# Layer 2's out-product with its operands swapped, tokens interleaved by four, and the coefficient set-up placed later

## The chip, the cores and the metric

The program runs on one core of one Trainium2 chip. The metric is the time of the device for one execution in microseconds, as the median of several; lower is better. The core has five engines that run their own instruction queues: TensorE (PE; its weight loads are listed apart as PEld), VectorE (DVE), ScalarE (ACT), GpSimd (POOL) and SyncE (SP), which issues most of the DMAs here.

## What is computed

A causal 7-tap filter over the sequence, and then two layers on 8192 tokens of 192 features, each with 2048 hidden units. The first has a relu6 gate, the second a rational activation.

```python
# x (2, 4096, 192); weight (8, 7); softmax over the taps of each head
out = np.einsum('hk,bskhg->bshg', softmax(weight), x_unf)      # filter
h = x @ w_in                                                   # layer 1
g = h * np.clip(h + 3.0, 0.0, 6.0) / 6.0
x = g @ w_out
h = x @ w_in                                                   # layer 2
P = a[0] + a[1] * h + a[2] * h2 + a[3] * h3
Q = 1.0 + np.abs(b[0]) * np.abs(h) + np.abs(b[1]) * h2
g = P / (Q + 1e-06)
return (g @ w_out).astype(np.float32)
```

## The kernel before

**Tiling.** Tokens are taken in 16 blocks (NB) of 512 (BLK), hidden units in 16 tiles of 128 (NF), which makes 256 tile steps (NT) per layer. Activations lie with features on the partitions: 192 features are a part "a" of 128 (DA) and a part "b" of 64 (DB). A tile step of a layer is an in-product (five matmuls that give h, 128 hidden units x 512 tokens, in one PSUM bank), elementwise work on VectorE, ScalarE and GpSimd that gives g, and an out-product (five matmuls that add g's share to the accumulators of the block).

**Split operands.** Matmuls use the rounded one-pass format fp32r. Every operand is held as a rounded high part and the rest, and a product is three: hi x hi, lo x hi, hi x lo. In `out_product` (L369 to 385) the weights w_out are the stationary operand and g the moving one with 512 columns: a_hi and a_lo on g_hi, a_hi on g_lo into `ya_acc` (L379 to 381), and a mixed operand b_hl, whose columns 0 to 63 are b's high part and 64 to 127 its low part, on g_hi and g_lo into `yb_acc` (L384, L385). Output rows are features, and `yb_acc` holds two halves that are added later.

**Order.** Every engine's queue is written out by `run` from hand-made plans (START, BEGIN, RAMP, MIDDLE, TURN, END): an entry is a stage, its lag in steps behind layer 1's step p or layer 2's step s, and for work of a block the step inside the block. Layer 2 starts 20 steps behind layer 1 (IN2). In the middle, a step has one layer-1 and one layer-2 tile, and TensorE's order is in1, in2, out1, out2.

**The end of a block in layer 2.** ScalarE scales `ya_acc` into `y_a` (y2a_out, L657) and the upper half of `yb_acc` into `y_b` (y2b_move, L664); VectorE adds the scaled lower half (y2b_sum, L669, for the last block also L675). The first out-product of the next block waits for these (`left` in `out_product`). `store_y` issues two DMAs, 256 and 128 KB, to an output laid out as features x batch x tokens; the host transposes it.

**The last tiles.** Nine of the last fifteen tiles (FULL) aren't split: their g and weights are plain fp32 (L433 and L434, two fp32 products that appear as two instructions each). Their weights, `w_full`, are loaded again by `load_w_full` from within `store_y` of block 14 into buffers that are no longer used. `spare_products` (L423) issues products whose result isn't used. From tile 236 on (DEEP) elementwise buffers are four deep and use, among others, columns 0 to 511 of `stage_w`.

**Set-up.** The activation is evaluated in a form that divides by the cubic coefficient. Eight VectorE operations on one column (`monic_...`, L949 to L978) prepare its constants; the START plan puts them behind layer 1's tiles 5 to 11, on VectorE's queue. The first num2 waits for all of them (MONIC_READY). Two PSUM banks of layer 2's accumulators serve as the buffer of layer 1's gate for the first 21 tiles (`gated`). WARM products on a tile of ones run before the first data is there (L1066).

Of the kernel before, what the change touches and what calls it, by code (L numbers as in the profile page):

```python
# [5 lines left out]
F32 = mybir.dt.float32  # L6
# [5 lines left out]
P = 128  # L12
# [37 lines left out]
    "vector": [("monic_side", 5), ("monic_safe", 6), ("monic_inverse", 7), ("monic_c2", 8), ("gate1", 0), ("monic_ratio", 9),  # L50
             ("monic_c01", 10), ("monic_scale", 11), ("conv_b1", AHEAD, (2, 2, 2, 3, 5, 6, 7), 1), ("g1lo", 1),
# [10 lines left out]
             ("x2b_res", SUM1, 0), ("g1lo", 1), ("x2b_lo", SUM1, 0), ("conv_a", AHEAD, (6, 4, 4, 16, 4, 5))],  # L62
# [15 lines left out]
    "scalar": [("y2b_move", SUM2, 0), ("y2a_out", SUM2, 0), ("cs_b_hi", AHEAD, 13, 0),  # L78
# [5 lines left out]
             ("cs_b_lo", AHEAD, 15, 0), ("y2b_sum", SUM2, 0), ("g_neg", 2), ("gate1", 0), ("newton", 1),  # L84
# [10 lines left out]
             ("y2b_move", SUM2, -3)],  # L95
    "vector": [("num2", 1), ("g_neg", 2), ("num1", 1), ("x2b_lo", SUM1, 8), ("newton", 1), ("g_first", 1),
             ("x2b_res", SUM1, 3), ("g2lo", 2), ("y2b_sum", SUM2, -2)],
# [7 lines left out]
             ("y2b_move", SUM2, 3)],  # L105
    "vector": [("num2", 1), ("y2b_sum", SUM2, 0), ("num1", 1), ("g_neg", 2), ("x2b_res", SUM1, -3), ("g2lo", 6),
# [22 lines left out]
def build_program(nc, x_a, x_b, taps, coefs, w_pack, out):  # L129
# [10 lines left out]
    assert n_batch == 2 and n_layers == 2 and DA + DB == out.shape[0] and DB * 2 == P  # L140
# [45 lines left out]
    with ExitStack() as ctx:  # L186
# [13 lines left out]
        WO = DA + P + DA  # L200
# [12 lines left out]
        y_a = [sb(f"y{l}_a", BLK) for l in range(2)]  # L213
        y2_b = sb("y2_b", BLK, F32, DB)
# [40 lines left out]
        ya_acc = [bank(f"y{l}a_acc") for l in range(2)]  # L255
        yb_acc = [bank(f"y{l}b_acc") for l in range(2)]

        yb_last = h_banks[bank2[NT - H_BANKS]][0:DB, :]
# [7 lines left out]
        def quotient(t):  # L266
            return ([ya_acc[0], yb_acc[0]][t % 2] if t >= SPARE else h_banks[bank2[t]])[:, :]
# [4 lines left out]
        spent = [r1[0], r1[1], y_a[0], raw_a[1], x2b_rest]  # L272
        w_full = {t: spent[i // 2][:, i % 2 * (DA + DB):(i % 2 + 1) * (DA + DB)] for i, t in enumerate(full)}
# [30 lines left out]
        def wait_buffer(eng, t, used, *others):  # L304
# [8 lines left out]
            else:  # L313
                eng.wait_ge(S[used], t - 3)
                if used == "g_first" and t - 4 in on_gpsimd:
# [6 lines left out]
        d_w_full = sem("d_w_full")  # L322
# [7 lines left out]
                   y2b_part y1a_out x2a_hi x2b_hi x2b_res x2a_lo x2b_lo  # L330
                   y2a_out y2b_move y2b_sum product_a product_b sum_p sum_v setup_v setup_s root ones""".split()
# [38 lines left out]
        def out_product(eng, l, t, g_hi, g_lo, left):  # L370

            k, f = divmod(t, NF)
            c = f * WO
            w = wout[l]
            first, last = f == 0, f == NF - 1
            a_hi, b_hl, a_lo = w[:, c:c + DA], w[:, c + DA:c + DA + P], w[:, c + DA + P:c + WO]
            if first:
                after(eng, S[left[0]], k)
            eng.matmul(ya_acc[l][:, :], a_hi, g_hi[:, :], start=first, stop=False)  # L379
            eng.matmul(ya_acc[l][:, :], a_lo, g_hi[:, :], start=False, stop=False)  # L380
            eng.matmul(ya_acc[l][:, :], a_hi, g_lo[:, :], start=False, stop=last)
            if first:
                after(eng, S[left[1]], k)
            eng.matmul(yb_acc[l][:, :], b_hl, g_hi[:, :], start=first, stop=False)  # L384
            return eng.matmul(yb_acc[l][:, :], b_hl, g_lo[:, :], start=False, stop=last)  # L385
# [20 lines left out]
        def pe_out1(eng, t):  # L406
            first_block_weights(eng, 0, t, "w_out_done")
            eng.wait_ge(S["g1lo"], t + 1)
            out_product(eng, 0, t, g1_hi[t % 2], g1_lo[t % 2], ("y1a_out", "x2b_lo")) \
                .then_inc(S["n1_done"], 1)  # L410
# [768 lines left out]
```

## Time and profile before

| | |
|---|---|
| median of 3 runs | 1202.07 us (1201.59 to 1202.16) |
| the profiled execution | 1204.0 us, its span 1201.9 us |
| granted TensorE clock, mean | 0.998 |
| TensorE / its weight loads | busy 1186.5 us (99%) / 963.2 us (80%) |
| VectorE | busy 1160.7 us (97%) |
| ScalarE / GpSimd | busy 1065.5 us (89%) / 1072.9 us (89%) |
| DMA | 22.02 MB, 18 GB/s over the span |

The span runs from the first to the last instruction of the program. A busy share is the union of an engine's instructions. Matmuls overlap in the records, so that their busy time says little about their pace: what counts is the time from one start to the next. "Idle before" is the time in which the engine did nothing ahead of a group, with the engine that released it.

### The profile page before, as it was taken

The numbers are of one execution on the slowest core, as the hardware profiler recorded it, in microseconds if no ns is written. First come the engines' busy times: TensorE is split into PE (matmuls) and PEld (weight loads), VectorE is DVE, ScalarE is ACT, GpSimd is POOL, SyncE is SP. The second block draws the span as 40 slices with busy tenths as digits, with TensorE's granted clock in tenths as the row PEclk, the third lists the DMA queues.
The fourth block names the chain that finished last, engine by engine and source line by source line (L and its number), as shares of the span: only waits on it lengthen the run. The fifth ranks groups of instructions, "written<-read, shape, count | busy, mean of one in ns | idle before, by whom it ended". The sixth has DMA issues, their size and how long they took to land. (4 is left out here: it accounts for less than half of the span.)

```text
span 1201.9 us, 17842 instructions
## 1 busy us (share of the span) xinstructions
PE 1186.5 (99%) x5145; PEld 963.2 (80%) x5145; DVE 1160.7 (97%) x1784; ACT 1065.5 (89%) x1980; POOL 1072.9 (89%) x829
## 2 busy tenths in 40 slices
PE   8999999999999999999999999999999999999998
PEld 6778888888888888888888888888888888888754
DVE  7999999999999999999999999999999999998898
ACT  7888899898998988989998899889999899888886
POOL 5989989898998989999898998999989899898874
PEclk9999999999999999999999999999999999999999
DMA  4400000000000000010000000000000000000010
GB/s 147 152 2 10 1 23 1 23 10 23 1 1 24 9 23 1 1 32 1 22 1 15 17 2 23 1 23 10 1 23 1 23 1 1 14 1 14 1 44 13
DMA packets 11313, 22.02 MB, mean 18 GB/s; under 512 B 1744, under 2 KB 3152, under 8 KB 11216
## 3 DMA queue, kind: packets, MB, share of 16 engines
q1 hardware_dynamic: 10928, 20.89, 5.9%
q8 instruction: 40, 0.66, 0.2%
q14 instruction: 57, 0.47, 0.1%
q10 hardware_dynamic: 288, 0.01, 0.0%
HBM read 14.60 MB, written 6.29 MB: 17 GB/s over the span
## 5 line engine op out<-in xcount | busy, mean ns | idle before, releaser
L525 POOL TENSOR_TENSOR den<-den,sqr 128x512 f32<-128x512 f32 x246 | 360.7, 1466 | 92.3 <-ACT den L499 91.1
L599 POOL TENSOR_TENSOR g_lo<-g,g_hi 128x512 fp32r<-128x512 f32 x246 | 319.4, 1298 | 7.9 <-ACT g_hi L605 7.9
L492 POOL TENSOR_TENSOR g_lo<-r,g_hi 128x512 fp32r<-128x512 f32 x235 | 309.9, 1319 | 1.7 <-ACT g_hi L605 1.3
L605 ACT ACTIVATE g_hi<-g 128x512 fp32r<-128x512 f32 x246 | 155.9, 634 | 54.9 <-PE y1b_acc L385 47.1
L529 ACT ACTIVATE rsq<-den 128x512 f32<-128x512 f32 x246 | 155.0, 630 | 45.6 <-POOL den L525 42.7
L519 DVE SCALAR_TENSOR_TENSOR num<-h,monic,num 128x512 f32<-128x512 f32 x246 | 184.6, 751 | 8.2
L513 DVE SCALAR_TENSOR_TENSOR num<-h,monic,sqr 128x512 f32<-128x512 f32 x246 | 183.2, 745 | 0.0
L552 DVE SCALAR_TENSOR_TENSOR h<-num,monic,h 128x512 f32<-128x512 f32 x238 | 178.3, 749 | 0.2
L478 DVE SCALAR_TENSOR_TENSOR r<-r,h 128x512 f32<-128x512 f32 x235 | 160.4, 683 | 14.2 <-ACT r L471 13.4
L545 DVE SCALAR_TENSOR_TENSOR den<-den,h 128x512 f32<-128x512 f32 x238 | 161.9, 680 | 1.0 <-ACT h L541 0.9
L574 DVE SCALAR_TENSOR_TENSOR g<-den,h 128x512 f32<-128x512 f32 x238 | 161.1, 677 | 0.2
L605 ACT ACTIVATE g_hi<-r 128x512 fp32r<-128x512 f32 x235 | 149.3, 635 | 8.7 <-issue 0.3
L471 ACT ACTIVATE r<-h 128x512 f32<-128x512 f32 x256 | 150.0, 586 | 5.9 <-DVE y1b_acc L478 2.5
L505 ACT ACTIVATE sqr<-h 128x512 f32<-128x512 f32 x246 | 145.2, 590 | 2.3
L541 ACT ACTIVATE h<-rsq 128x512 f32<-128x512 f32 x240 | 143.2, 597 | 4.4 <-DVE num L519 3.5
L499 ACT ACTIVATE den<-h 128x512 f32<-128x512 f32 x246 | 146.1, 594 | 0.0
L367 PE MATMUL h<-x0a_hi,win_hi 128*128 128x512 f32 x256 | 100.5, 393 | 2.3 <-DVE r L478 1.2
L379 PE MATMUL y0a_acc<-g_hi,wout 128*128 128x512 f32 x256 | 100.3, 392 | 2.3 <-DVE g_lo L492 1.6
L367 PE MATMUL h<-x1a_hi,win_hi 128*128 128x512 f32 x256 | 100.6, 393 | 0.1
L367 PE MATMUL h<-x0b_hl,win_hi 128*128 128x512 f32 x256 | 100.5, 393 | 0.0
L367 PE MATMUL h<-x1a_lo,win_hi 128*128 128x512 f32 x256 | 99.9, 390 | 0.6 <-POOL x1a_lo L613 0.6
L367 PE MATMUL h<-x0a_lo,win_hi 128*128 128x512 f32 x256 | 99.8, 391 | 0.6 <-DVE x0a_lo L611 0.6
(182 smaller groups left out, 2886.8 us busy)
## 6 DMA issues: line engine op xcount, KB each, us to landing
stage_w<-w_pack SPq DMA_DIRECT2D x16, 448.0 KB, 3.4
raw_a<-x_a SPq DMA_DIRECT2D x16, 259.0 KB, 3.2
out<-y_a SPq DMA_DIRECT2D x16, 256.0 KB, 2.0
out<-y_b SPq DMA_DIRECT2D x16, 128.0 KB, 2.3
raw_b<-x_b SPq DMA_DIRECT2D x14, 129.5 KB, 2.7
r<-w_pack SPq DMA_DIRECT2D x4, 96.0 KB, 2.0
raw_b<-x_b SPq DMA_DIRECT2D x4, 65.5 KB, 4.6
y_a<-w_pack SPq DMA_DIRECT2D x2, 96.0 KB, 2.3
```

The source lines that it names most:

```text
L367: mm = eng.matmul(psum, w, x[:, :], start=(i == 0), stop=(i == len(passes) - 1))
L478: eng.scalar_tensor_tensor(out=gated(t)[:, :], in0=r1[t % 2][:, :], scalar=1.0, in1=h1_of(t), op0=ALU.min, op1=ALU.mult).then_inc(S["gate1 ...
L492: eng.tensor_tensor(g1_lo[t % 2][:, :], gated(t)[:, :], f32(g1_hi[t % 2][:, :]), ALU.subtract).then_inc(S["g1lo"], 1)
L513: eng.scalar_tensor_tensor(out=num_of(t), in0=h2_of(t), scalar=c2, in1=sqr_of(t), op0=ALU.add, op1=ALU.mult).then_inc(S["num2"], 1)
L519: eng.scalar_tensor_tensor(out=n, in0=h2_of(t), scalar=c1, in1=n, op0=ALU.mult, op1=ALU.add).then_inc(S["num1"], 1)
L525: eng.tensor_tensor(den_of(t), den_of(t), sqr_of(t), ALU.add).then_inc(S["den_sum"], 1)
L529: eng.activation(rsq[t % 2][:, :], den_of(t), ACT.Abs_reciprocal_sqrt, bias=Q_ONE).then_inc(S["rsq_done"], 1)
L545: eng.scalar_tensor_tensor(out=den_of(t), in0=den_of(t), scalar=Q_ONE, in1=quotient(t), op0=ALU.add, op1=ALU.mult).then_inc(S["newton"], 1)
L552: eng.scalar_tensor_tensor(out=raw_quotient(t), in0=num_of(t), scalar=c0, in1=quotient(t), op0=ALU.add, op1=ALU.mult).then_inc(S["g_first" ...
L574: eng.scalar_tensor_tensor(out=g2[t % 2][:, :], in0=den_of(t), scalar=2.0, in1=raw_quotient(t), op0=ALU.subtract, op1=ALU.mult) \
L599: eng.tensor_tensor(g2_lo[t % 2][:, :], g2[t % 2][:, :], f32(g2_hi[t % 2][:, :]), ALU.subtract).then_inc(S["g2lo"], 1)
L605: return eng.activation(dst, src, ACT.Copy)
```

## The change

Layer 1 stays as it is. In layer 2's out-product the operands change places: g is the stationary operand, in four groups of 128 tokens, and w_out the moving one with 192 columns (D), so that output rows are tokens. A group takes every fourth token of the block (`tokens(i)`), and so partition p holds the tokens 4p to 4p + 3; two groups share a PSUM bank. A tile has 12 matmuls: per group w_hi and w_lo on g_hi, and w_hi on g_lo. Unsplit tiles have four fp32 products. `wout[1]` now holds w_hi and w_lo side by side, 384 columns a tile as before. Each bank is emptied by one scaled copy of 128 x 384; y2b_sum and the addition of halves are gone, and for the last block the second copy is on VectorE. The output is laid out as batch x tokens x features, and a store's rows are two tokens, 1536 bytes. Six of the nine unsplit weights go to free columns of `stage_w` (512 to 895), and are loaded one block earlier. The eight set-up operations move from the START plan (steps 5 to 11) to the BEGIN plan (steps 12 to 18). num2 and g_neg wait for the same events in another order.

```diff
 START = {
-    "vector": [("monic_side", 5), ("monic_safe", 6), ("monic_inverse", 7), ("monic_c2", 8), ("gate1", 0), ("monic_ratio", 9),
-             ("monic_c01", 10), ("monic_scale", 11), ("conv_b1", AHEAD, (2, 2, 2, 3, 5, 6, 7), 1), ("g1lo", 1),
+    "vector": [("gate1", 0), ("conv_b1", AHEAD, (2, 2, 2, 3, 5, 6, 7), 1), ("g1lo", 1),
 BEGIN = {
-             ("x2b_res", SUM1, 0), ("g1lo", 1), ("x2b_lo", SUM1, 0), ("conv_a", AHEAD, (6, 4, 4, 16, 4, 5))],
+             ("x2b_res", SUM1, 0), ("g1lo", 1), ("x2b_lo", SUM1, 0), ("conv_a", AHEAD, (6, 4, 4, 16, 4, 5)),
+             ("monic_side", 12), ("monic_safe", 13), ("monic_inverse", 14), ("monic_c2", 15), ("monic_ratio", 16),
+             ("monic_c01", 17), ("monic_scale", 18)],
 MIDDLE = {
-    "scalar": [("y2b_move", SUM2, 0), ("y2a_out", SUM2, 0), ("cs_b_hi", AHEAD, 13, 0),
+    "scalar": [("y2b_out", SUM2, 0), ("y2a_out", SUM2, 0), ("cs_b_hi", AHEAD, 13, 0),
-             ("cs_b_lo", AHEAD, 15, 0), ("y2b_sum", SUM2, 0), ("g_neg", 2), ("gate1", 0), ("newton", 1),
+             ("cs_b_lo", AHEAD, 15, 0), ("g_neg", 2), ("gate1", 0), ("newton", 1),
...
-        spent = [r1[0], r1[1], y_a[0], raw_a[1], x2b_rest]
-        w_full = {t: spent[i // 2][:, i % 2 * (DA + DB):(i % 2 + 1) * (DA + DB)] for i, t in enumerate(full)}
+        spent = [st[:, BLK:BLK + 2 * D] for st in stage_w] + [r1[0], r1[1], y1_a, raw_a[1], x2b_rest]
+        w_full = {t: spent[i // 2][:, i % 2 * D:(i % 2 + 1) * D] for i, t in enumerate(full)}
+        in_stage = full[:2 * W_STAGES]
...
+        def tokens(i):
+            return slice(i, BLK, BLK // P)
+
+        def y2_of(i):
+            return y2_acc[i // 2][:, i % 2 * D:(i % 2 + 1) * D]
+
+        def out_product2_hi(eng, t):
+            k, f = divmod(t, NF)
+            w, g_hi = wout[1][:, f * WO:(f + 1) * WO], g2_hi[t % 2]
+            for i in range(BLK // P):
+                y, g = y2_of(i), g_hi[:, tokens(i)]
+                if f == 0 and i % 2 == 0:
+                    after(eng, S[("y2a_out", "y2b_out")[i // 2]], k)
+                eng.matmul(y, g, w[:, 0:D], start=f == 0 and i % 2 == 0, stop=False, skip_group_check=True)
+                eng.matmul(y, g, w[:, D:WO], start=False, stop=False, skip_group_check=True)
+
+        def out_product2_lo(eng, t, groups):
+            f = t % NF
+            for i in groups:
+                ins = eng.matmul(y2_of(i), g2_lo[t % 2][:, tokens(i)], wout[1][:, f * WO:f * WO + D],
+                                 start=False, stop=f == NF - 1, skip_group_check=True)
+            return ins
...
             if t in full:
-                eng.wait_ge(d_w_full, 16 * len(full))
                 wait_g(eng, t)
-                w, g = w_full[t], g2[t % 2][:, :]
-                eng.matmul(ya_acc[1][:, :], w[:, 0:DA], g, start=False, stop=False)
-                eng.matmul(yb_acc[1][0:DB, :], w[:, DA:DA + DB], g, start=False, stop=False) \
-                    .then_inc(S["n2_done"], 1)
+                if t in in_stage:
+                    eng.wait_ge(d_w_stage, 16 * len(in_stage))
+                else:
+                    eng.wait_ge(d_w_full, 16 * (len(full) - len(in_stage)))
+                for i in range(BLK // P):
+                    ins = eng.matmul(y2_of(i), g2[t % 2][:, tokens(i)], w_full[t], start=False, stop=False,
+                                     skip_group_check=True)
+                ins.then_inc(S["n2_done"], 1)
             if t < NT - 2:
                 eng.wait_ge(S["g2lo"], splits(t))
-                out_product(eng, 1, t, g2_hi[t % 2], g2_lo[t % 2], ("y2a_out", "y2b_sum")) \
-                    .then_inc(S["n2_done"], 1)
+                out_product2_hi(eng, t)
+                out_product2_lo(eng, t, range(4)).then_inc(S["n2_done"], 1)
...
+        def y2_half(half):
+            return y2[:, half * 2 * D:(half + 1) * 2 * D]
-            eng.activation(y_a[1][:, :], ya_acc[1][:, :], ACT.Copy, scale=minus_scale).then_inc(S["y2a_out"], 1)
+            eng.activation(y2_half(0), y2_acc[0][:, 0:2 * D], ACT.Copy, scale=minus_scale).then_inc(S["y2a_out"], 1)
...
-        def y2b_sum(eng, k):
+        def y2b_out(eng, k):
+            if (k == NB - 1) != (eng is nc.vector):
+                return
+            eng.wait_ge(S["n2_done"], (k + 1) * NF)
             after(eng, d_out_b, 16 * k)
+            scaled(eng, y2_half(1), y2_acc[1][:, 0:2 * D], minus_scale).then_inc(S["y2b_out"], 1)
...
         def w_out_lo(eng, c):
+            if c >= n_chunks:
+                minus(eng, wo[:, :, D:WO], raw_out, f32(wo[:, :, 0:D])).then_inc(S["w_out_done"], 1)
+                return
...
         def store_y(eng, k):
+            if k == NB - 3:
+                load_w_full(eng, in_stage, d_w_stage, ("w_in_done", 2 * n_chunks), ("w_out_done", 2 * n_chunks))
             if k == NB - 2:
-                load_w_full(eng)
+                load_w_full(eng, full[len(in_stage):], d_w_full, ("g1lo", NT), ("x2a_lo", NB),
+                            ("conv_a_tap", K * NB), ("x2b_lo", NB))
+            rows = out[k % 2, bass.ds(k // 2 * BLK, BLK), :].rearrange("(p g) d -> p g d", p=P)
+            for half, name, landed in ((0, "y2a_out", d_out_a), (1, "y2b_out", d_out_b)):
+                eng.wait_ge(S[name], k + 1)
+                eng.dma_start(rows[:, 2 * half:2 * half + 2, :],
+                              y2_half(half).rearrange("p (g d) -> p g d", d=D)).then_inc(landed, 16)
```

## Rows read from the trace of the kernel before

**Rows 1.** The page's first part: busy time, share of the span, instructions.
```profile
PE 1186.5 (99%) x5145; PEld 963.2 (80%) x5145; DVE 1160.7 (97%) x1784; ACT 1065.5 (89%) x1980; POOL 1072.9 (89%) x829
```
**Rows 2.** Stages: length, then PE, PEld, DVE, ACT, POOL busy, clock, DMA share, GB/s.
```profile
100.00:1139.00 1039.00, 1039.00 (x4584) 860.36 (x4583) 1013.29 (x1550) 934.38 (x1724) 953.82 (x717) 1.00 0.04 11
...
1139.00:1202.00 63.00, 55.46 (x184) 30.51 (x182) 58.84 (x91) 47.34 (x88) 40.23 (x32) 0.99 0.09 27
```
**Rows 3.** Timeline of TensorE about 600 us: start and length in us, engine, line.
```profile
599.77 0.39 PE L379 MATMUL y0a_acc<-g_hi,wout 128*128 128x512 f32 x1
...
600.90 0.39 PE L379 MATMUL y1a_acc<-g_hi,wout 128*128 128x512 f32 x1
...
604.30 0.39 PE L379 MATMUL y0a_acc<-g_hi,wout 128*128 128x512 f32 x1
```
**Rows 4.** Products into layer 2's accumulator up to 1139 us: ns, first and last start.
```profile
L379 PE MATMUL y1a_acc<-g_hi,wout x236: 388/390/390, 79.3 to 1138.2; 128*128 128x512 f32 x118
```
**Rows 5.** Groups of TensorE's warm-up: count, busy us, mean ns of one, idle before.
```profile
L1066 PEld LDWEIGHTS h<-x1a_hi 128*128 128x128 f32 x21 | 4.7, 244 | 3.5 <-POOL x1a_hi L1128 2.4
...
L1066 PE MATMUL h<-x1a_hi 128*128 128x512 f32 x15 | 5.2, 518 | 2.4 <-POOL x1a_hi L1128 2.4
L1066 PE MATMUL h<-x1a_hi 128*128 128x256 f32 x6 | 0.9, 282 | 0.0
...
L434 PEld LDWEIGHTS y1b_acc<-g,r 128*64 128x64 f32 x8 | 0.8, 134 | 3.0 <-issue 3.0
```
**Rows 6.** Timeline of TensorE's weight loads that come after an idle time.
```profile
10.15 0.19 PEld L367 LDWEIGHTS h<-x0a_hi,win_hi 128*128 128x128 f32 x1 [1.31 <-POOL win_lo L613]
10.26 0.19 PEld L367 LDWEIGHTS h<-x0a_hi,win_lo 128*128 128x128 f32 x1
...
1156.39 0.19 PEld L434 LDWEIGHTS y1b_acc<-g,r 128*64 128x64 f32 x2 [0.76 <-issue]
```
**Rows 7.** Timeline of TensorE at 8.4 us: three products in one row.
```profile
8.17 0.52 PE L1066 MATMUL h<-x1a_hi 128*128 128x256 f32 x3
```
**Rows 8.** Groups of ScalarE: scaled copies of 512 and of 256 columns.
```profile
L657 ACT ACTIVATE y_a<-y1a_acc,monic 128x512 f32<-128x512 f32 x16 | 11.0, 689 | 0.9 <-PE y1a_acc L458 0.6
L772 ACT ACTIVATE conv_a<-raw_a,tap 128x512 f32<-128x512 f32 x15 | 10.6, 710 | 0.0
L772 ACT ACTIVATE num<-raw_b,tap_ab 128x256 f32<-128x256 f32 x4 | 1.7, 494 | 0.0
```
**Rows 9.** Timeline of TensorE at 1153 us, with its idle time before.
```profile
1153.08 0.47 PE L379 MATMUL y1a_acc<-g_hi,wout 128*128 128x512 f32 x1 [0.45 <-ACT y_a L657]
```
**Rows 10.** A group of VectorE from 100 to 1139 us.
```profile
L669 DVE SCALAR_TENSOR_TENSOR y_b<-y1b_acc,monic,y_b 64x512 f32<-64x512 f32 x14 | 10.3, 733 | 0.8 <-ACT y_b L664 0.8
```
**Rows 11.** Timeline of VectorE and TensorE from 20 to 60 us.
```profile
34.18 1.24 DVE L968 TENSOR_TENSOR monic<-coef,monic 128x1 f32<-128x1 f32 x1
...
57.02 0.47 PE L379 MATMUL y0a_acc<-g_hi,wout 128*128 128x512 f32 x1 [0.60 <-ACT y_a L619]
...
58.35 0.50 PE L384 MATMUL y0b_acc<-g_hi,wout 128*128 128x512 f32 x1 [0.39 <-DVE x1b_hl L645]
```
**Rows 12.** Timeline of TensorE at an unsplit tile: each fp32 product is two instructions.
```profile
1155.45 1.02 PE L433 MATMUL y1a_acc<-g,r 128*128 128x512 f32 x2
1156.39 1.07 PE L434 MATMUL y1b_acc<-g,r 128*64 128x512 f32 x2
1157.40 0.50 PE L367 MATMUL h<-x1a_hi,win_hi 128*128 128x512 f32 x1
```
**Rows 13.** DMA issues: count, KB each, median us from issue to landing.
```profile
out<-y_a SPq DMA_DIRECT2D x16, 256.0 KB, 2.0
...
r<-w_pack SPq DMA_DIRECT2D x4, 96.0 KB, 2.0
```
**Rows 14.** Timeline of the last VectorE operation and the last store.
```profile
1198.40 0.74 DVE L675 SCALAR_TENSOR_TENSOR y_b<-h,monic,y_b 64x512 f32<-64x512 f32 x1 [0.32 <-PE h L460]
...
1199.17 0.47 SPq L897 DMA_DIRECT2D out<-y_b  x1
```

More of the change, by code:

```diff
@@ L104 @@
              ("x2b_hi", SUM1, -10), ("sq2", 0), ("rec2", 1), ("y2a_out", SUM2, 2), ("g2hi", 2),
-             ("y2b_move", SUM2, 3)],
-    "vector": [("num2", 1), ("y2b_sum", SUM2, 0), ("num1", 1), ("g_neg", 2), ("x2b_res", SUM1, -3), ("g2lo", 6),
+             ("y2b_out", SUM2, 3)],
+    "vector": [("num2", 1), ("num1", 1), ("g_neg", 2), ("x2b_res", SUM1, -3), ("g2lo", 6),
              ("x2b_lo", SUM1, -2), ("newton", 1), ("g_first", 1)],
@@ L139, in build_program @@
     XW, HW = BLK + K - 1, HALF + K - 1
-    assert n_batch == 2 and n_layers == 2 and DA + DB == out.shape[0] and DB * 2 == P
+    assert n_batch == 2 and n_layers == 2 and DA + DB == out.shape[2] and DB * 2 == P
     assert SPARE == NT - NF
@@ L210, in build_program @@
         conv_a, conv_b = sb("conv_a", BLK), sb("conv_b", BLK)
-        y_a = [sb(f"y{l}_a", BLK) for l in range(2)]
-        y2_b = sb("y2_b", BLK, F32, DB)
+        y1_a = sb("y1_a", BLK)
+        y2 = sb("y2", BLK // P * D)
         x2b_rest = sb("x2b_rest", BLK)
@@ L329, in build_program @@
                    conv_a_tap conv_b_tap cs_a_hi cs_b_half cs_b_hi cs_a_lo cs_b_lo
-                   y2b_part y1a_out x2a_hi x2b_hi x2b_res x2a_lo x2b_lo
-                   y2a_out y2b_move y2b_sum product_a product_b sum_p sum_v setup_v setup_s root ones""".split()
+                   y1a_out x2a_hi x2b_hi x2b_res x2a_lo x2b_lo
+                   y2a_out y2b_out product_a product_b sum_p sum_v setup_v setup_s root ones""".split()
         S = {n: sem(n) for n in names}
@@ L368, in in_product, with out_product1 @@
             return mm
-        def out_product(eng, l, t, g_hi, g_lo, left):
+        def out_product1(eng, t, g_hi, g_lo):
             k, f = divmod(t, NF)
-            c = f * WO
-            w = wout[l]
+            w = wout[0][:, f * WO:(f + 1) * WO]
             first, last = f == 0, f == NF - 1
-            a_hi, b_hl, a_lo = w[:, c:c + DA], w[:, c + DA:c + DA + P], w[:, c + DA + P:c + WO]
+            a_hi, b_hl, a_lo = w[:, 0:DA], w[:, DA:DA + P], w[:, DA + P:WO]
             if first:
[L378 to L381, printed above, removed]
+                after(eng, S["y1a_out"], k)
+            eng.matmul(y1a_acc[:, :], a_hi, g_hi[:, :], start=first, stop=False)
+            eng.matmul(y1a_acc[:, :], a_lo, g_hi[:, :], start=False, stop=False)
+            eng.matmul(y1a_acc[:, :], a_hi, g_lo[:, :], start=False, stop=last)
@@ L382, in out_product @@
             if first:
-                after(eng, S[left[1]], k)
-            eng.matmul(yb_acc[l][:, :], b_hl, g_hi[:, :], start=first, stop=False)
-            return eng.matmul(yb_acc[l][:, :], b_hl, g_lo[:, :], start=False, stop=last)
+                after(eng, S["x2b_lo"], k)
+            eng.matmul(y1b_acc[:, :], b_hl, g_hi[:, :], start=first, stop=False)
+            return eng.matmul(y1b_acc[:, :], b_hl, g_lo[:, :], start=False, stop=last)
+        def tokens(i):
+            return slice(i, BLK, BLK // P)
@@ L618, in y1a_out @@
             after(eng, S["x2a_lo"], k)
[L619 removed]
+            eng.activation(y1_a[:, :], y1a_acc[:, :], ACT.Copy).then_inc(S["y1a_out"], 1)
         def x2a_hi(eng, k):
```

100 lines of the change are left out of this document (35 added, 65 removed).

## The prediction

> **What bounds the kernel now.** I read the busy shares first [rows 1]: TensorE is busy 99% of the span, VectorE 97%, and the rest are near 89%. A busy TensorE isn't yet a full one, because its matmuls overlap, so the next view is the table of stages [rows 2]. From 100 to 1139 us TensorE is never idle, at a granted clock of 1.00 (its level of 2.4 GHz), while VectorE has 26 of 1039 us free, ScalarE 105 and GpSimd 85. The timeline decides [rows 3]: one step's out-products of layer 1 begin at 599.77, layer 2's at 600.90, and the next step's at 604.30. So a step of 20 products takes 4.53 us, and one product 226.6 ns from start to start. Of these 512/2.4 = 213.3 ns are columns and 13.3 ns come on top. The group of layer 2's out-products [rows 4] shows 236 of them started between 79.3 and 1138.2 us, with almost no idle time before them. So whatever one layer-2 tile takes more or less on TensorE is paid 236 times, as long as VectorE keeps up. Before 79 us no out-product of layer 2 runs, and after 1139 us TensorE waits for the elementwise engines now and then [rows 2].
>
> **Step 1, the out-product of layer 2.** Removed are 5 products of 512 columns: 5 x 226.6 = 1133 ns. Added are 12 products of 192 columns (four token groups, each with w_hi and w_lo on g_hi, and w_hi on g_lo). Columns fall from 2560 to 2304, which alone would be worth 107 ns a tile. But each product needs its own stationary operand, and now that is 128 columns of g. Does a repeated operand get loaded again? The warm-up products all use the same `ones`, and still each has its load: 21 loads for 15 + 6 products with full operands [rows 5]. So 12 loads per tile instead of 5.
>
> What is the price of a load that nothing long covers? Two loads behind an idle array start 0.11 us apart (10.15 and 10.26) [rows 6]. Of a pair with 64 columns the union is 0.19 us; less the 0.134 of one such load [rows 5] this leaves 0.055 us. Both are 0.85 ns a column, 109 ns for 128, whatever streams. The other end is the shortest product that the trace has in this number format, 256 columns: three of them have a union of 0.52 us [rows 7]; less the 0.282 of one [rows 5] they start 0.12 us apart. That is 256/2.4 + 13.3 = 120 ns too, so it doesn't tell whether the load or the stream set it. For 192 columns the stream asks for 80 + 13.3 = 93 ns, less than a load. So the load decides: between 109 ns (loads alone) and 120 ns (a load beside a product). The two rows are equally near, one having the load that binds and no stream, the other the stream and a load that may not bind; I take the middle, 114.5 ns. 12 x 114.5 = 1374 ns, +241 ns a tile; 236 x 241 = **+56.9 us**. The ends: 12 x 109 = 1308, +175, +41.2 us; 12 x 120 = 1440, +307, +72.3 us.
>
> The new operand is read with a step of four words, from every fourth token. No TensorE row of this trace has a step, so I bound it by the plain load (109 ns, no change; a gain has no reason, since a column still has to be fetched for each token) and by a load twice as long. I take no change, because the moving operand is fetched at 2.4 columns per ns [rows 3] and a load at 128/109 = 1.2, so half the port's rate would do. The other end is rival B.
>
> **Step 2, emptying the banks.** ScalarE's copies shrink from 512 columns (y_a, 689 ns) to 384. A scaled copy of 128x512 takes 710 and of 128x256 takes 494 ns, 0.84 ns a column [rows 8], so about 580 ns each. TensorE meets its waits for them 15 products, 3.4 us, after the block's last one; today only one such wait shows, 0.45 us at 1153.08 [rows 9]. Behind it on TensorE's queue stand the rest of the tile and the next in-product, but the copies now end earlier, so nothing is added. VectorE loses y2b_sum, 733 ns a block, 10.3 us in the long stretch [rows 10]. It isn't the bound there, so this is worth nothing now; it would matter only if TensorE got faster (rival C).
>
> **Step 3, set-up later.** Eight one-column VectorE operations leave the stretch from 26 to 42 us; the longest takes 1.24 us [rows 11], the others far less. In that stretch TensorE hardly waits, so leaving it gains nothing. They go behind tiles 12 to 18 (about 47 to 62 us), where TensorE does wait for VectorE's x1b_hl: 0.39 us at 58.35, after 0.60 for ScalarE's y_a at 57.02 [rows 11]. Queued behind them on VectorE are the next tile's gate1 and g1lo, for which ScalarE and TensorE wait. Bounds: -0.2 us to +1.5 us (all of them in front of that wait); I take +0.3, one or two of them. num2 of tile 0 waits for all eight; it is placed three steps after the last of them. num2 and g_neg wait for the same events as before in another order, which costs nothing where the last event stays the last.
>
> **Step 4, the last tiles.** The nine tiles with unsplit weights go from two fp32 products (128 and 64 columns stationary, 512 moving) to four of 192 moving. Each is two instructions. Today 1155.45 to 1156.39 to 1157.40 [rows 12]: 0.94 and 1.01 us, that is 2 x 0.427 of stream, some 0.09 that isn't overlapped, and a load. With 192: 2 x 0.16 + 0.09 + 0.11 = 0.52, times four 2.1 us against 2.05. No difference. The ten split tiles there cost 0.24 us more each, where the critical chain passes mostly through VectorE, GpSimd and only at the end through TensorE; I take +0.5 us of 2.4 (bounds 0 and 2.4). Loading six of the nine weights a block earlier moves DMAs of 96 KB, about 2 us each [rows 13], on SP's queue behind the store of block 12, ahead of block 13's. SP then waits only for the end of weight preparation, long past. Nothing. w_out_lo of layer 2 becomes one GpSimd operation of the same columns instead of two, in the ramp; TensorE waits there for other things [rows 11]: nothing.
>
> **Step 5, the end.** Today the last product starts at about 1197.9, then L675 takes 0.74 us and its store is issued at 1199.17 [rows 14]. After: 12 products by 114.5 instead of 7 by 230, -0.2 us, and a copy of 384 columns on VectorE, -0.1 us. Stores of 192 KB in rows of 1536 bytes replace 256 and 128 KB, about 2 us to land either way [rows 13]. In all -0.3 us.
>
> **Sum.** +56.9 + 0.3 + 0.5 - 0.3 = +57.4 us. The profiled span is 1201.9 us and that execution took 1204.0, 1.9 above the median of 1202.07; the difference applies to the median: 1202.1 + 57.4 = **1259.5 us**. With the ends of step 1 and the small terms: 1243 to 1278.
>
> **The rivals.** B, **the stepped load is slower.** If fetching every fourth word halves a load's rate, a load takes 218 ns and sets the pace: 12 x 218 = 2616, +1483 ns, x 236 = +350 us; in the last tiles out- and in-product (2616 + 1133 ns, 3.75 us) then also pass VectorE's pace (58.8 us for the last 16 tiles [rows 2]), some +3 us: 1555 us. The Trainium skill states this danger: "SBUF — State Buffer", in the note on cachelines under "Door 1", says that reads are at full rate while they hit the same 16-byte line at least twice, and that crossing to a new line each time costs. Here each column would be a new line. By that rule this rival holds, without it the sum above; no row here has such a read. For it: nothing in the trace excludes it. Against it: a load runs at half the stream's rate, so the port has room. Chance 0.15. A third size is that short products themselves have a price: at the unsplit fp32 products' 0.86 us per 512 columns [rows 12], 322 ns for 192, it would be +2.9 us a tile, 1880 us. Chance 0.03.
>
> C, **faster: the stream decides, not the load.** If a load can be hidden below 94.4 ns (1133/12), the sign turns. At 93.3 ns: 12 x 93.3 = 1120, -13 ns, x 236 = -3.2: 1199 us. If the 13.3 ns also go, 12 x 80 = 960 ns, VectorE becomes the bound: of 1039 us it needs 1013.3 - 10.3 = 1003, -36 us: 1166 us. The Trainium skill, "TensorE: Matmul & The Clock Gate", section "Back-to-back issue gap", gives N/2.4 + 2.5 ns, 82.5 ns here, which would be this case; the trace's 226.6 ns for 512 columns already lies above that rule. Against both: the pairs of loads at 0.11 us [rows 6], and that repeated operands are loaded again [rows 5]. Chances 0.08 and 0.02.
>
> **How the numbers follow.** Forecast (loads set the pace) 0.72, B 0.15, the still slower one 0.03, C 0.08 and 0.02. The range takes the forecast's own 1243 to 1278, rounded out to 1280, and C's first case, 1197: 0.80. A measurement tells about 0.2% (2.4 us). Faster: 0.02 + 0.05 of C; same: 0.03 of C, where the gain is under 2.4 us; slower: 0.90.
>
> **What would show it.** Twelve products per layer-2 tile, 0.11 to 0.12 us from start to start in the timeline, each with a load that starts when the product before it does; a step of 4.77 us; the weight-load row busy nearly without gap in the out-product; VectorE down to about 92% in the long stretch; clock still 1.00. Loads of 0.3 us and a spacing of 0.2 us or more show B. A spacing under 0.094 us shows C. A wait before the first product of a block would say that step 2 is wrong, and gaps beyond 1.5 us around 58 us that step 3 is.

## The result

| | time, median | range | executions |
|---|---|---|---|
| before | 1202.12 us | 1201.59 to 1202.17 | 4 |
| changed kernel | 1583.17 us | 1583.05 to 1584.69 | 4 |

The changed kernel is slower by a factor of 1.317 (95% interval 1.3153 to 1.3187), +381 us. The forecast was 1259.5 us, with a range of 1197 to 1280. The direction held and the size didn't: the nearest of the prediction's cases is rival B, priced at 1555 us.

The profile of the changed kernel begins with its span and busy shares (compare [rows 1]). Its chain of waits follows.

```profile
span 1581.4 us, 21343 instructions
...
PE 1569.4 (99%) x6908; PEld 1422.0 (90%) x6908; DVE 1166.5 (74%) x1768; ACT 1081.6 (68%) x1979; POOL 1047.7 (66%) x821
...
PE 96%; DVE 2%; ACT 1%; issue 1%; DMA 0%; POOL 0%; DVEq 0%; ACTq 0%
```

VectorE, ScalarE and GpSimd are busy for nearly as many microseconds as before, but now these are only 66 to 74% of the span. TensorE is 96% of the chain that ended last. The stages (columns as in [rows 2]; the second one begins here where tile 235's num2 does) show it as well:

```profile
100.00:1489.00 1389.00, 1389.00 (x6144) 1263.75 (x6143) 1011.31 (x1524) 944.24 (x1710) 923.87 (x712) 1.00 0.03 9
1489.00:1581.40 92.40, 89.31 (x393) 84.41 (x391) 70.49 (x108) 58.70 (x110) 52.47 (x41) 0.98 0.04 12
```

In the long stretch TensorE never idles, as before, and its granted clock is 1.00, as before. So the time is neither a wait nor the clock. It is in the products themselves, as the timeline of TensorE over one step shows (compare [rows 3]):

```profile
799.96 0.39 PE L382 MATMUL y1a_acc<-g_hi,wout 128*128 128x512 f32 x1
...
801.10 0.25 PE L405 MATMUL y_acc<-wout,g_hi 128*128 128x192 f32 x1
801.19 0.39 PE L406 MATMUL y_acc<-wout,g_hi 128*128 128x192 f32 x1
801.42 0.40 PE L405 MATMUL y_acc<-wout,g_hi 128*128 128x192 f32 x1
...
802.83 1.10 PE L411 MATMUL y_acc<-wout,g_lo 128*128 128x192 f32 x4
803.77 0.42 PE L371 MATMUL h<-x0a_hi,win_hi 128*128 128x512 f32 x1
...
806.07 0.39 PE L382 MATMUL y1a_acc<-g_hi,wout 128*128 128x512 f32 x1
```

A step takes 6.11 us (799.96 to 806.07) instead of 4.53. The 512-column products are still 0.23 us apart. The products of 192 columns are 0.23 to 0.24 us apart too, though they stream only 80 ns worth of columns. Layer 2's out-product takes 2.67 us (801.10 to 803.77) instead of 1.13. The weight loads in the same place:

```profile
801.31 0.33 PEld L405 LDWEIGHTS y_acc<-wout,g_hi 128*128 128x128 f32 x1
801.55 0.33 PEld L406 LDWEIGHTS y_acc<-wout,g_hi 128*128 128x128 f32 x1
...
803.79 0.19 PEld L371 LDWEIGHTS h<-x0a_hi,win_lo 128*128 128x128 f32 x1
```

The loads of g, read with a step of four words, take 0.33 us each and start 0.235 us apart. A load of plain weights (L371) takes 0.19. The next load starts before the last has ended, so it is the distance of the starts that counts: each product starts when its load lets it, 12 times a tile.

The theory after the result is therefore: the load of the stepped operand costs 235 ns where a plain one should cost 109 to 120 (the prediction's bounds), and nothing else of the change matters much. Its rivals: swapped products of 192 columns are slow by themselves, whatever the layout of g; or the set-up or the last tiles hold part of the 381 us. Three experiments each undo or do one part. The others measure how a step acts on the load and on the stream, since the prediction's argument was about the room between those two.

### The profile page after: what moved, and what is told of

It is laid out like the page before. It is cut to its first block, busy times and chain, and to the rows that moved or that the text cites. A ratio compares the mean times of both kernels' runs of the same rounds, so it can differ in the third digit from the quotient of the medians.

```text
span 1581.4 us, 21343 instructions
## 1 busy us (share of the span) xinstructions
PE 1569.4 (99%) x6908; PEld 1422.0 (90%) x6908; DVE 1166.5 (74%) x1768; ACT 1081.6 (68%) x1979; POOL 1047.7 (66%) x821
## 4 chain that ended last, share of the span: by engine, by line
PE 96%; DVE 2%; ACT 1%; issue 1%; DMA 0%; POOL 0%; DVEq 0%; ACTq 0%
PE h L371 36%; PE y_acc L406 15%; PE y_acc L411 15%; PE y_acc L405 12%; PE y1b_acc L388 4%; PE y1a_acc L382 4%; PE y1a_acc L384 3%; PE y1b_acc L387 3%; PE y1a_acc L383 3%; PE y_acc L463 1%; DVE y_acc L497 0%; DVE g_lo L511 0%; ACT r L490 0%; DMA tap_ab<-taps 0%; DVE y1a_acc L721 0%
## 5 line engine op out<-in xcount | busy, mean ns | idle before, releaser
L544 POOL TENSOR_TENSOR den<-den,sqr 128x512 f32<-128x512 f32 x246 | 334.4, 1359 | 325.9 <-ACT den L518 325.1
L406 PE MATMUL y_acc<-wout,g_hi 128*128 128x192 f32 x988 | 391.9, 397 | 0.0
L405 PE MATMUL y_acc<-wout,g_hi 128*128 128x192 f32 x988 | 356.8, 361 | 0.1
L405 PEld LDWEIGHTS y_acc<-wout,g_hi 128*128 128x128 f32 x988 | 321.9, 326 | 10.0 <-issue 0.5
L406 PEld LDWEIGHTS y_acc<-wout,g_hi 128*128 128x128 f32 x988 | 321.9, 326 | 0.0
L511 POOL TENSOR_TENSOR g_lo<-r,g_hi 128x512 fp32r<-128x512 f32 x235 | 302.9, 1289 | 12.4 <-ACT g_hi L625 11.9
L411 PE MATMUL y_acc<-wout,g_lo 128*128 128x192 f32 x988 | 272.7, 398 | 0.0
L411 PEld LDWEIGHTS y_acc<-wout,g_lo 128*128 128x128 f32 x988 | 256.0, 332 | 0.0
```

Source lines behind the costliest of these rows:

```text
L405: eng.matmul(y, g, w[:, 0:D], start=f == 0 and i % 2 == 0, stop=False, skip_group_check=True)
L406: eng.matmul(y, g, w[:, D:WO], start=False, stop=False, skip_group_check=True)
L411: ins = eng.matmul(y2_of(i), g2_lo[t % 2][:, tokens(i)], wout[1][:, f * WO:f * WO + D], start=False, stop=f == NF - 1, skip_group_check=True)
L511: eng.tensor_tensor(g1_lo[t % 2][:, :], gated(t)[:, :], f32(g1_hi[t % 2][:, :]), ALU.subtract).then_inc(S["g1lo"], 1)
L544: eng.tensor_tensor(den_of(t), den_of(t), sqr_of(t), ALU.add).then_inc(S["den_sum"], 1)
```

## The experiments

**The swapped products without the step.** Token groups become 128 neighbouring tokens; the number and size of products, the copies and the set-up stay as in the changed kernel. The store has to follow: its rows are 768 bytes.

```diff
-            return slice(i, BLK, BLK // P)
+            return slice(i * P, (i + 1) * P)
...
-            rows = out[k % 2, bass.ds(k // 2 * BLK, BLK), :].rearrange("(p g) d -> p g d", p=P)
+            rows = out[k % 2, bass.ds(k // 2 * BLK, BLK), :].rearrange("(g p) d -> p g d", p=P)
```

> The changed kernel, but a group is 128 tokens side by side instead of every fourth, so that the stationary operand is read without a step; the store's rows are then 768 bytes. Theory S (the step is what made a load 235 ns): the 12 loads of a tile cost 109 to 120 ns each, a step of the middle is 4.71 to 4.84 us, the time 1244 to 1278 us, 1259 at 114.5 ns. Rival T (a load that only a 192-column product covers costs 235 ns whatever its step): 1583 us as the changed kernel. Rival U (the stores' short rows matter): would show as waits of ScalarE for the store, over 1583 us.

Measured: 1255.10 us (1254.79 to 1255.52), 1.0442 of before (interval 1.0426 to 1.0458; before was 1201.75 beside it). TensorE's products and its loads:

```profile
803.12 0.28 PE L406 MATMUL y_acc<-wout,g_hi 128*128 128x192 f32 x1
803.23 0.28 PE L405 MATMUL y_acc<-wout,g_hi 128*128 128x192 f32 x1
803.34 0.27 PE L406 MATMUL y_acc<-wout,g_hi 128*128 128x192 f32 x1
```
```profile
803.14 0.19 PEld L405 LDWEIGHTS y_acc<-wout,g_hi 128*128 128x128 f32 x1
803.25 0.19 PEld L406 LDWEIGHTS y_acc<-wout,g_hi 128*128 128x128 f32 x1
```

One edit takes 328 us away. Loads of 0.19 us start 0.11 us apart (111 to 112 ns over a tile) and a step takes 4.753 us (mean of the steps from 700 to 900 us). No copy out of the accumulators waits for a store, so the shorter rows of the output play no part. So the stepped read holds 328 of the 381 us. What is left, +53 us, is the change as the prediction saw it, forecast at +57.4. Short products are not slow by themselves.

**Load or stream?** The same kernel with half the columns per product: the plain kernel's spacing of 112 ns might be that of the 192 columns and not of the load. Half of layer 2's output is left out.

```diff
-                eng.matmul(y, g, w[:, 0:D], start=f == 0 and i % 2 == 0, stop=False, skip_group_check=True)
-                eng.matmul(y, g, w[:, D:WO], start=False, stop=False, skip_group_check=True)
+                eng.matmul(y[:, 0:D // 2], g, w[:, 0:D // 2], start=f == 0 and i % 2 == 0, stop=False, skip_group_check=True)
+                eng.matmul(y[:, 0:D // 2], g, w[:, D:D + D // 2], start=False, stop=False, skip_group_check=True)
```

> As the kernel with plain tokens, but each split product of layer 2 streams 96 of its 192 columns, so that half of layer 2's output is left out. Loads are the same in number and size. If the load sets the pace, nothing moves: the spacing and the time are those of the plain kernel within 5 us. If the stream or the 13.3 ns beyond it still count beside the load, the spacing falls by up to 40 ns, 12 x 40 x 236 = 113 us.

```profile
803.02 0.27 PE L406 MATMUL y_acc<-wout,g_hi 128*128 128x96 f32 x1
803.13 0.27 PE L405 MATMUL y_acc<-wout,g_hi 128*128 128x96 f32 x1
803.24 0.28 PE L406 MATMUL y_acc<-wout,g_hi 128*128 128x96 f32 x1
```

96 columns, 40 ns of stream, still 0.11 us from start to start, 112 ns over a tile. The load sets the pace. The time itself, 1262.75 us in one execution, is 7.7 us above the full columns' 1255.10 and so misses the 5 us that were expected. The profiled spans are 7.2 us apart. Of these, 1.7 us arise before tile 8 (the granted clock is 0.83 from 10 to 20 us, 1.00 in the plain kernel), 4.6 in the long stretch, where the products of layer 2's in-product are 229 ns apart instead of 227, and 0.9 at the end. Why the 512-column products were slower is open. Nothing here got faster with the columns halved, and the spacing is what answers the question.

**A step of two words.** Each group takes every second token of 256; output rows are still 1536 bytes.

```diff
-            return slice(i, BLK, BLK // P)
+            return slice(i // 2 * 2 * P + i % 2, (i // 2 + 1) * 2 * P, 2)
...
-            rows = out[k % 2, bass.ds(k // 2 * BLK, BLK), :].rearrange("(p g) d -> p g d", p=P)
+            rows = out[k % 2, bass.ds(k // 2 * BLK, BLK), :].rearrange("(h p g) d -> p h g d", p=P, g=2)
```

> The changed kernel, but a group takes every second token of a half block, so that two columns of a load lie in each 16-byte line and the output rows stay at 1536 bytes. Theory S1 (two hits on a line are enough for the full rate): the same as with plain tokens, 1244 to 1278 us. Theory S2 (each new line costs; the loads' time is linear in their lines, 114.5 ns for 32 lines, 235 for 128): 64 lines give 155 ns a load, 12 x 155 = 1860 ns a tile, +727 x 236 = +172, 1374 us. Rival T: 1583 us.

Measured: 1277.43 us (1277.23 to 1277.5), 1.0629 (1.0612 to 1.0645).

```profile
802.75 0.20 PEld L405 LDWEIGHTS y_acc<-wout,g_hi 128*128 128x128 f32 x1
802.87 0.20 PEld L406 LDWEIGHTS y_acc<-wout,g_hi 128*128 128x128 f32 x1
802.99 0.20 PEld L405 LDWEIGHTS y_acc<-wout,g_hi 128*128 128x128 f32 x1
```

118 to 120 ns from start to start, only 6 to 8 more than without a step. A price that rises in a straight line from step one to step four would give 112 + 123/3 = 153 ns and some 1370 us, and falls. What fits is a load paid by the 16-byte lines it touches (the lines of rival B): step two touches 64 of them, 118/64 = 1.84 ns a line, and step four 128, 235/128 = 1.84. Of the 22 us over plain groups, eleven loads a tile at 6.5 ns explain some 17; the rest goes with 512-column products that are 229 ns apart here instead of 227.

**A step of three words**, which touches 96 lines, tells a price by lines from one that jumps at "one word a line". Layer 2's outputs are those of other tokens.

```diff
-            return slice(i, BLK, BLK // P)
+            return slice(i, i + 3 * P - 2, 3)
```

> The changed kernel with a step of three words in the stationary reads (columns i, i + 3, ... of g), so that the outputs of layer 2 are those of other tokens; only the time counts. 128 columns then lie on 96 lines of 16 bytes. Theory S3 (a load takes the longer of 0.85 ns a column and some 1.8 ns a line: 235 ns for 128 lines, 118 for 64): 96 lines give 170 to 176 ns, 12 x 173 = 2076 ns, +0.96 us x 236, 1430 us. Rival (only a step of a full line is slow, everything under it is nearly free): 118 to 125 ns a load, 1277 to 1300 us. Rival (any step above two is as slow): 235 ns, 1583 us.

Measured: 1431.67 us, in one execution.

```profile
800.03 0.26 PEld L405 LDWEIGHTS y_acc<-wout,g_hi 128*128 128x128 f32 x1
800.20 0.26 PEld L406 LDWEIGHTS y_acc<-wout,g_hi 128*128 128x128 f32 x1
800.38 0.26 PEld L405 LDWEIGHTS y_acc<-wout,g_hi 128*128 128x128 f32 x1
```

176 ns a load, 176/96 = 1.83 ns a line. So for 128 columns of this format the four layouts fit the larger of 0.87 ns a column (112) and 1.84 ns a line (118, 176, 235).

A rival fits the same four times: the larger of 112 ns and 59 ns for each word of step (118, 176, 235), whatever the lines. Up to a step of four words 128 columns touch 32 lines for each word of step, so the two can't be told apart. A step of eight would do it, with 128 lines still: 235 ns by lines, 470 ns by words of step. It wasn't run. That the line is the unit is therefore argued, and what is shown is the price of the four steps.

**Does the stream pay as well?** The prediction argued with room: the moving operand is fetched twice as fast as a load, so a load at half the port's rate would do. If that were the right picture, a step of two should cost the stream as little as it costs the load. In the plain kernel, x of layer 2 is read with a step, in-product only; the accumulator is written in the same order.

```diff
+                moving, to = x[:, :], psum
+                if l == 1:
+                    moving = moving.rearrange("p (c s) -> p s c", s=4)
+                    to = to.rearrange("p (s c) -> p s c", s=4)
+                mm = eng.matmul(to, w, moving, start=(i == 0), stop=(i == len(passes) - 1))
```

> The kernel with plain token groups, but layer 2's in-product streams its tokens with a step of four words (x viewed as 128 x 4), so that h and g come out reordered and the output rows are those of the changed kernel. All loads are plain; the moving operand is what has the step. If the argument of my prediction holds (the stream's port has room at a load's rate), a stepped stream must show that room: free would be 1255 us. If the stream pays 0.83 ns a line (half its column rate): 440 ns a product instead of 227, +1.07 us a tile, 1510 us. If it pays the load's price of 1.8 ns a line: 920 ns a product, +3.5 us a tile, 2080 us, and there was never any room.

> The same with a step of two words, two columns to a line. Free or half rate as above: 1255 to 1262 us, since two hits on a line keep up. If the stream pays 1.8 ns a line: 256 lines give 460 ns a product, +1.17 us a tile, 1530 us.

Measured, one execution each: step four 1546.15 us, step two (s=2) 1536.95 us. Timeline of TensorE with step four:

```profile
806.32 0.64 PE L375 MATMUL h<-x1a_hi,win_lo 128*128 128x512 f32 x1
806.78 0.64 PE L375 MATMUL h<-x1a_lo,win_hi 128*128 128x512 f32 x1
```

and with step two:

```profile
807.03 0.61 PE L375 MATMUL h<-x1a_hi,win_hi 128*128 128x512 f32 x1
807.47 0.63 PE L375 MATMUL h<-x1a_hi,win_lo 128*128 128x512 f32 x1
```

0.46 and 0.45 us a product instead of 0.227, 0.90 and 0.88 ns a column. For step four that is half the rate, as expected of one word a line: 0.90 ns a line, where the load of the same layout pays 1.84. The 1255 to 1262 us expected of step two were missed by 275 us: two words a line don't save the stream. Either any step halves it, or it is something else in this form, such as an operand made of several runs.

**Step two as one run.** Each in-product of layer 2 becomes two products of 256 columns, every one a single stepped run.

```diff
+                for h in range(2):
+                    mm = eng.matmul(psum[:, h * HALF:(h + 1) * HALF], w, x[:, h:BLK:2],
+                                    start=(i == 0 and h == 0), stop=last, skip_group_check=True)
```

> The kernel with plain token groups; each in-product of layer 2 is two products of 256 columns, the even and the odd tokens, each read in one run with a step of two words (the earlier stepped streams were read in two or four runs). Theory V (any step halves the stream's rate, 0.9 ns a column, whether two columns or one lie on a line): 230 to 240 ns per product of 256, ten of them 2.35 us instead of 1.13, about 1545 us. Rival W (it was the several runs that cost, a step of two is free): 120 ns each, 1.2 us, 1271 us.

**Runs without a step.** The same products of 256 columns, now as four pieces of 64 neighbouring columns, in place of the stepped slice (layer 2's rows come out in another order).

```diff
-                    mm = eng.matmul(psum[:, h * HALF:(h + 1) * HALF], w, x[:, h:BLK:2],
+                    mm = eng.matmul(psum[:, h * HALF:(h + 1) * HALF].rearrange("p (a b) -> p a b", b=DB), w, x[:, :].rearrange("p (a b) -> p a b", b=P)[:, :, h * DB:(h + 1) * DB],
```

> The same with two products of 256 columns, each read as four pieces of 64 columns side by side, without a step; layer 2's rows come out in another order. Theory V: pieces are free, 120 ns a product, 1271 us. Rival W (pieces cost): over 200 ns a product, 1500 us or more.

Measured, one execution each: 1549.26 us with the step, 1276.75 us with the pieces. Timelines of TensorE, first with the step, then with the pieces; each line is two products:

```profile
802.25 0.65 PE L376 MATMUL h<-x1a_hi,win_lo 128*128 128x256 f32 x2
802.72 0.64 PE L376 MATMUL h<-x1a_lo,win_hi 128*128 128x256 f32 x2
```
```profile
800.59 0.40 PE L376 MATMUL h<-x1a_hi,win_lo 128*128 128x256 f32 x2
800.83 0.40 PE L376 MATMUL h<-x1a_lo,win_hi 128*128 128x256 f32 x2
```

0.47 us for a stepped pair and 0.24 us for a pair in pieces (the times expected were 1545 and 1271 us). 120 ns a product is also what [rows 7] gave for contiguous ones. So it is the step between neighbouring columns that halves the stream, not the number of pieces.

**Only the set-up later.** The kernel before, with nothing changed but the place of the eight `monic` operations on VectorE.

```diff
-    "vector": [("monic_side", 5), ("monic_safe", 6), ("monic_inverse", 7), ("monic_c2", 8), ("gate1", 0), ("monic_ratio", 9),
-             ("monic_c01", 10), ("monic_scale", 11), ...
+    "vector": [("gate1", 0), ...
...
+             ("monic_side", 12), ("monic_safe", 13), ("monic_inverse", 14), ("monic_c2", 15), ("monic_ratio", 16),
+             ("monic_c01", 17), ("monic_scale", 18)],
```

> The kernel before with the eight set-up operations moved to steps 12 to 18 and nothing else changed. My term of the sum: +0.3 us with bounds -0.2 and +1.5, so 1201.9 to 1203.6 us; TensorE's waits about 57 and 58 us (0.60 and 0.39) grow by what is added. Rival: leaving VectorE's full stretch from 26 to 42 us gains up to 2 us, 1200 us.

Measured: 1205.51 us (1205.05 to 1208.17), 1.0038 (1.0024 to 1.0052), +3.8 us over the 1201.75 us of before beside it, and so more than the upper bound of step 3. The counterpart is the plain-token kernel with the set-up back in its old place, by the same edit reversed:

> The kernel with plain token groups and the set-up operations back at steps 5 to 11. Theory: the 3.8 us that the later set-up cost the kernel before (TensorE's wait for x1b_hl of 2.4 us and half the clock for about 3 us after it) are in this kernel too, so it takes 1251.3 us, within 1250.8 to 1252.5, and TensorE's wait at 58 us is 0.4 us again. Rival (a slower layer 2 absorbs it): 1255 us.

Measured: 1253.21 us (1252.36 to 1254.9), 1.0421 (1.0404 to 1.0439; before was 1202.79 beside it). That is +50.4 us over before, against +53.4 with the set-up late: 2.9 us less. The two intervals overlap, so this pair alone proves little, but both pairs point the same way. The timelines of TensorE in this pair show the mechanism. First the set-up early:

```profile
55.31 0.47 PE L381 MATMUL y1a_acc<-g_hi,wout 128*128 128x512 f32 x1 [0.60 <-ACT y_a L638]
...
56.42 0.50 PE L386 MATMUL y1b_acc<-g_hi,wout 128*128 128x512 f32 x1 [0.18 <-DVE x1b_hl L664]
...
57.48 0.39 PE L370 MATMUL h<-x0a_hi,win_lo 128*128 128x512 f32 x1
57.71 0.39 PE L370 MATMUL h<-x0a_lo,win_hi 128*128 128x512 f32 x1
```

then late:

```profile
54.81 0.47 PE L382 MATMUL y1a_acc<-g_hi,wout 128*128 128x512 f32 x1 [0.60 <-ACT y_a L639]
...
57.93 0.50 PE L387 MATMUL y1b_acc<-g_hi,wout 128*128 128x512 f32 x1 [2.19 <-DVE x1b_hl L665]
...
59.24 0.63 PE L371 MATMUL h<-x0a_hi,win_lo 128*128 128x512 f32 x1
59.67 0.63 PE L371 MATMUL h<-x0a_lo,win_hi 128*128 128x512 f32 x1
```

and VectorE with the set-up late:

```profile
54.02 1.08 DVE L991 SCALAR_TENSOR_TENSOR monic<-coef,monic 128x1 f32<-128x1 f32 x2
...
57.18 0.69 DVE L665 TENSOR_TENSOR x1b_hl<-x2b_rest,y1b_acc 64x512 fp32r<-64x512 f32 x1
```

The `monic` operations in front of x1b_hl (1.08 us here for two, 0.90 us at 48.4, 0.14 at 50.4) make it start at 57.18 instead of 55.67. TensorE, which comes 0.5 us earlier here (54.81 instead of 55.31), waits 2.19 us for it instead of 0.18, and goes on 1.5 us later (57.93 instead of 56.42). And after that wait its products are 0.43 us apart instead of 0.23: the granted clock is at its lower level of 1.2 GHz for some 3 us. The stages from 50 to 60 and 60 to 70 us give 0.96 and 0.87 with the set-up late:

```profile
50.00:60.00 10.00, 7.02 (x27) 4.90 (x26) 9.21 (x16) 7.05 (x15) 6.56 (x6) 0.96 0.45 146
60.00:70.00 10.00, 10.00 (x40) 8.09 (x39) 8.55 (x14) 7.40 (x14) 5.18 (x4) 0.87 0.00 0
```

and 1.00 in both with it early. 0.87 over 10 us is 1.3 us lost, 0.96 another 0.4. With the 1.5 us by which TensorE goes on later this makes 3.2 us, and tile 8's num2 starts 3.2 us later too (100.35 instead of 97.18). The medians give 2.9 in this pair and 3.8 with the old products.

The kernel before can't be laid beside its late version in the same way. In its profiled execution the clock was 0.83 from 10 to 20 us, where it was 1.00 in the late version's, so TensorE comes to this place about 2 us late: the product that waits for x1b_hl starts at 58.35 in it and at 58.32 with the set-up late. That execution's span is 1201.9 us, those of the nine beside the late version 1199.3 to 1200.1.

No version here beats the kernel before. The best with swapped operands is the one with plain token groups and the set-up early, 1253.21 us.

## Why the prediction was wrong, point by point

**What bounds the kernel: right.** TensorE sets the pace, and each step's surplus is paid 236 times, less a few. From tile 8 to tile 235 the start of num2 moves from 98.3 and 1125.0 us to 105.8 and 1489.3: 1383.5 us instead of 1026.7, 1.57 us for each of 227 tiles. Up to tile 8 the added work is 7.4 us, partly hidden in other waits.

**Step 1: the count right, one price wrong.** Each product has its own load, also where the operand repeats: L405, L406 and L411 have 988 products and as many loads each. The plain load was put at 114.5 ns between 109 and 120; it took 112. The forecast of a 4.77 us step is 4.753 us in the plain-token kernel. The step that failed is the paragraph after it: the stepped read was put at no cost, because the moving operand is fetched at twice a load's rate, so that "half the port's rate would do". It costs 235 - 112 = 123 ns a load. From num2 of tile 8 to that of tile 235 the changed kernel takes 1383.5 us and the plain-token one 1076.3: 1.353 us for each of 227 tiles, which is eleven times 123 ns, since a tile's first load runs beside a product of 512 columns. So 307 of the 328 us lie there, 5 before it and 15 behind it. The argument took the stream's rate as a measure of what a load's reads can do. With a step of four the stream still takes a column every 0.90 ns, nearly the rate of a plain load (0.87), so the room that the argument saw is there for the stream; the load of the same layout takes 1.84 ns a column. And at a step of two the stream has halved (0.88 ns a column) where the load is almost untouched (118 ns). Neither rate tells of the other.

With plain groups the sum came close: +53.3 us (1255.10 against 1201.75) for +57.4. The difference is mostly the load, 112 ns for 114.5; the set-up's 3 us, forecast at 0.3, made up for part of it.

**Rival B: the stepped load right, with 218 ns for 235.** It had a chance of 0.15, and the argument that outweighed it rested on no row with a stepped read. Its +1.48 us a tile was +1.57. The Trainium skill, "SBUF — State Buffer", note on cachelines under "Door 1", says that reads run at full rate while they hit the same 16-byte line at least twice. For loads this case nearly agrees: 118 ns at two words a line against 112, 235 at one. For the stream it doesn't: two words a line still gave 451 ns for 512 columns instead of 227, and there the measurement decides. That the line is what a load pays for stays argued, as said above.

**The third size and rival C: not met.** The third size is also summed wrongly: 12 x 322 ns less 1133 is +2.7 us a tile and some 1850 us, not +2.9 and 1880; those come out only with 13.3 ns a product on top. In C, the formula of the Trainium skill's "TensorE: Matmul & The Clock Gate", section "Back-to-back issue gap", is by that section itself one for an isolated product, and counts too little at small N where every product has its load. It was no support for a faster case, and the spacing here was 112 ns, not 82.5.

**Step 2: right.** The copy of 384 columns takes 565 to 582 ns, about 580 as estimated, and no product in the long stretch waits for a bank. The last two copies:

```profile
1577.94 0.58 ACT L680 ACTIVATE y<-y_acc,monic 128x384 f32<-128x384 f32 x1 [4.70 <-PE y_acc L411]
1578.42 0.62 DVE L785 TENSOR_SCALAR y<-y_acc,monic 128x384 f32<-128x384 f32 x1 [4.28 <-PE y_acc L411]
```

In the plain-token kernel VectorE is busy 977 of 1039 us, 94%, where 92% was said.

**Step 3: the place right, the size wrong.** x1b_hl is where it hurts, but +3.8 us instead of +0.3, beyond the bound of +1.5. "One or two of them" in front of the wait was too few: four stood there within 9 us (0.90, 0.14 and two of together 1.08 us), about 2 us, less 0.5 us that TensorE was earlier. And the clock was not priced at all: a wait of 2.2 us is followed by some 3 us at the lower level, which costs 1.7 us.

**Step 4: the sum right for plain loads by luck, small for stepped ones.** An unsplit tile's layer-2 out-product was put at 2.1 us against 2.05 before. Before it was 1.95 by [rows 12] (1155.45 to 1157.40). With plain groups it is 1.2 us from start to start, and with stepped ones 1.66. First plain, then stepped (the durations hold the last product's tail):

```profile
1243.89 1.46 PE L463 MATMUL y_acc<-r,g 128*128 128x192 f32 x8
...
1245.06 0.76 PE L450 MATMUL h<-win_hi,wout 128*128 128x512 f32 x2
```
```profile
1567.92 1.96 PE L463 MATMUL y_acc<-r,g 128*128 128x192 f32 x8
...
1569.58 0.99 PE L450 MATMUL h<-win_hi,wout 128*128 128x512 f32 x3
```

So the nine unsplit tiles take 0.75 us less of TensorE each instead of nothing less, and eleven tiles there are split, not ten. The plain fp32 loads take 190 ns each, the stepped ones 330, as with the other format.

From the start of tile 235's num2 to the end of the span it was 76.8 us before, 77.0 in the plain-token kernel (+0.2; +0.5 was forecast), and 92.1 in the changed one: +15.3, where rival B had +3. TensorE, which waited in this part before [rows 2], is now busy 89.3 of 92.4 us. The plain kernel gains nothing from its shorter unsplit tiles, since other engines set its pace there: VectorE is busy 19.9 of the 20 us from 1220 to 1240. Rival B took only the excess of a split tile's products over VectorE's pace; TensorE's whole sum for the part against its old time would have been the measure.

**Step 5: the size fits, but nothing tests it alone.** From the start of the last operation on the accumulators to the end of the span it was 3.5 us before (from 1198.40), 3.4 with plain groups (from 1250.27) and 3.0 in the changed kernel (from 1578.42). The last store is issued at 1579.06, 2.3 us before the end; before it was 2.7 us.

**The sum again.** Stepped loads 328 us (1583.17 against 1255.10); plain swapped products about 50 (1253.21 against 1202.79 with the set-up early); set-up late 3 to 4. Together 381.

What stays open: whether the load is paid by lines or by words of step, and why the stream is slowed by the smallest step and no more by a larger one. Both rest on few points in one number format, the step of three and all stepped streams on one execution each. A stepped load without products beside it wasn't tried. That TensorE's clock fell because of the wait is argued from the order of rows (set-up early: no long wait and no fall about 58 us; late: both), not from a run that has the wait alone. The fall from 12.5 us on in the kernel before fits it: TensorE had waited 1.10 us and 0.61 us just ahead of it. In the plain kernel with the set-up early these waits were 0.44 and 0.59 us, and the clock stayed up.

## What to carry to other kernels

In this number format, price a swapped product by its loads: count them (one per product, repeated operands too) and compare 112 ns per 128 columns with the columns that stream; here 192 columns couldn't cover a load, and 12 x 112 = 1344 ns was more than the 1133 ns it replaced even in the best layout. Keep both operands of a matmul contiguous, and get long output rows elsewhere: by a step of two words in the stationary operand at most, which cost 22 us here, where a step of four cost 328. Small operations moved into the queue of an engine that another waits for can cost more than their length: here about 2 us of them cost some 3, half of it through TensorE's clock. And where a price isn't in the trace and a rule speaks against it, weigh the rule by what it would cost, not by an argument of room.

## What the runs showed of the hardware

- Loads of 128 stationary fp32r columns, beside products of 192: the next one starts after 112 ns with neighbouring words, 118 to 120 ns with a step of two, 176 of three, 235 of four.
- A moving fp32r operand of 512 columns takes 227 ns contiguous, 451 ns with a step of two and 460 ns with a step of four (means over a stretch of the trace); pieces of 64 neighbouring columns cost nothing (120 ns for 256).
- Products of 192 and of 96 columns with loads of their own are equally far apart, 112 ns.
- After a wait of TensorE of 2.2 us, its 512-column products were 427 ns apart, the granted clock at its lower level, for about 3 us.
- Loads of the unsplit fp32 tiles took 190 ns each plain and 330 with a step of four.
